# Two steps of TensorE's hand-written order moved in front of their neighbours: the state's half of a 64-row chunk's output, and one group of transposes of batch 0

## The chip, the cores and the metric

The kernel runs on one core of one Trainium2 chip. The metric is the device time of one execution in microseconds (us). The core's engines work side by side, each on its own queue of instructions: TensorE (PE in the profile, its weight loads are PEld), VectorE (DVE), ScalarE (ACT), GpSimd (POOL) and SyncE (SP), which here only starts DMAs. They are ordered against each other only by semaphores on which the kernel waits.

## The reference

Three layers follow each other. The first is an attention with a decay in place of a softmax, over 4 batches, 8 heads, 576 positions and 64 features a head; the second a feed-forward layer over the 2304 rows; the third a mixture of 8 experts, of which each row takes two. Only the first layer has to do with the change.

```python
scores = scale * np.matmul(q, k.transpose(0, 1, 3, 2))
gamma = 1.0 - 2.0 ** (-5.0 - np.arange(H, dtype=np.float32))
rel = pos[:, None] - pos[None, :]
Dmat = np.where(rel >= 0, gamma[:, None, None] ** rel[None, :, :], 0.0)
ret = scores * Dmat[None, :, :, :]
attn_out = np.matmul(ret, v)
x = attn_out.transpose(0, 2, 1, 3).reshape(B * S, H * D)
x = _moe_ref(x=x, **moe_kwargs)           # softplus(x @ w_in) @ w_out
return _moe2_ref(x=x, **moe2_kwargs)      # top-2 of 8 experts
```

## The kernel before

The 576 positions of a batch are cut into five chunks (CHUNKS), four of 128 rows and a last one of 64 (ROWS). Since the decay is a power, a chunk's output has two parts: its own scores times its values, and what all earlier chunks of the batch have left in a state (64 x 64 a head) times its queries, which are scaled by a power of the decay. The first chunk of a batch has no second part. The work of a chunk t of batch b is:

- transpose_k (L623, four instructions, one a pair of heads): TensorE turns the chunk's keys into one of three PSUM banks; keep_kT (ScalarE, L955) copies them to kTb. It waits for the keys' DMA.
- scores (L637): TensorE multiplies keys and queries into the two score banks, of which there is only one set, so it waits until both masks of the chunk before are done (scores_masked). mask_scores (VectorE, L1215, two instructions, one a bank) multiplies them by the decay and writes them to sco.
- output: first the state's part (L656; it waits for x_kept, state_kept and q_scaled), then its own part (L663; it waits for scores_masked and the values' DMA), into the same two PSUM banks. Where the chunk has 64 rows, TensorE waits between the two parts until the first has been written (x_begun). keep_x (ScalarE, L961) copies the result away (x_kept).
- add_state (L676): TensorE multiplies keys and values; VectorE adds the faded old state (L1229, or a copy, L1231, for the first chunk) and raises state_kept. The last chunk of a batch has no add_state.
- scale_k (GpSimd, L507) scales the keys once they are turned, scale_q (GpSimd, L513) the queries once their scores are made (q_scaled). For each chunk GpSimd runs scale_k of the next one and then scale_q.

Each engine's order is written out by hand. TensorE's is that of the function sequence: for chunk t it turns the keys of chunk t+1, makes the scores of t, then the output and the state of t-1. So at t = 0 of a batch it turns chunk 1's keys, makes the scores of chunk 0, and then the output of the 64-row chunk of the batch before. Batch 0 starts with its own list of steps; batches 1 and 2 run in a loop. VectorE's order is: masks of t, fade of the state (L1221), add_state of t-1. In the last batch it also rounds off pieces of the feed-forward weights (piece_rest, L1234), after t = 1, 3 and 4, and ScalarE splits them (L947). After the last batch TensorE runs ff_in(0, 0) (L712 to L714, 12 matmuls in three kinds), the output of the last batch's 64-row chunk, and ff_in(0, 1), and goes on with the feed-forward layer.

A wait written with the function alone is an instruction of its own:

```python
def alone(eng, s, count):
    if not (isinstance(count, int) and count <= 0):
        eng.wait_ge(s, count)
        eng.sem_inc(passed, 1)
```

Of the kernel before, what the change touches and what calls it, by code (L numbers as in the profile page):

```python
# [27 lines left out]
P = 128  # L28
B, H, S, DH = 4, 8, 576, 64
# [3 lines left out]
CHUNKS = -(-S // P)  # L33
ROWS = [min(P, S - t * P) for t in range(CHUNKS)]
# [71 lines left out]
def build(nc, qT, kN, vN, w_ff, w_gn, noise, w_ex, c_q, c_k, c_dec, c_sq, c_small, c_pad, out):  # L106
    with ExitStack() as ctx:
        def sem(name):
            return ctx.enter_context(nc.semaphore(name))

        def place(name, shape, dt, at):
            at = -(-at // 32) * 32
            n = 4
            for s in shape[1:]:
                n *= s
            assert BASE <= at and at + n <= nc.sbuf_usable_end, (name, at, n)
            return nc.alloc_sbuf_tensor_at(name, shape, dt, offset=at), at + n
# [16 lines left out]
        vbuf, a = place("vbuf", [P, CHUNKS, D], F32, a)  # L134
# [3 lines left out]
        state, a = place("state", [P, 2, PAIRS, DH], F32, a)  # L138
# [109 lines left out]
        x_ps = x_banks[:, :, 0:2 * P].rearrange("p e (u c) -> p e u c", u=2)  # L248
# [22 lines left out]
        ld_v = [sem(f"ld_v{t}") for t in range(CHUNKS)]  # L271
# [6 lines left out]
        scores_made, scores_masked = sem("scores_made"), sem("scores_masked")  # L278
        x_begun, x_made, x_kept = sem("x_begun"), sem("x_made"), sem("x_kept")
# [30 lines left out]
        def at_least(eng, s, count):  # L310
# [10 lines that stand above are left out]
# [10 lines left out]
        def q_of(t):  # L331

            return qbuf[:, t, 0:PAIRS * ROWS[t]].rearrange("p (h s) -> p h s", h=PAIRS)
# [272 lines left out]
        def _(pe):  # L606


            def fill(n):
                for _ in range(n):  # L610
                    pe.matmul(gate_ps[:, 0:P], zero[:, :], zero[:, :], start=True, stop=True)
# [6 lines left out]
            def transpose_k(b, t):  # L618
                r, n = ROWS[t], b * CHUNKS + t
                pe.wait_ge(ld_k[t], b * 16 + 16)  # L620
                alone(pe, kT_kept, n - BACK[t] + 1)
                for h in range(PAIRS):
                    last = pe.transpose(kT_ps[t % 3][:, h, 0:r], kbuf[0:r, t, h * P:(h + 1) * P],  # L623
                                        ident[0:r, 0:r])
                last.then_inc(kT_made, 1)

            def scores(b, t):

                r, n = ROWS[t], b * CHUNKS + t
                pe.wait_ge(kT_kept, n + 1)  # L630
                alone(pe, ld_q[t], b * 16 + 16)
                alone(pe, scores_masked, n * 2)
                q = q_of(t)
                for h in range(PAIRS):
                    for e in range(2):
                        d = slice(e * DH, (e + 1) * DH)
                        last = pe.matmul(sc_ps[e][0:r, h, 0:r], kTb[d, t % 3, h, 0:r], q[d, h, :],  # L637
                                         start=True, stop=True)
                        if h == PAIRS - 1:
                            last.then_inc(scores_made, 1)  # L640

            def output(b, t):

                r, n = ROWS[t], b * CHUNKS + t
                pe.wait_ge(scores_masked, n * 2 + 2)
                alone(pe, ld_v[t], b * 16 + 16)
                at_least(pe, x_kept, n)
                at = lambda h, e: x_ps[(h + e) % 2 * DH:((h + e) % 2 + 1) * DH, e, h // 2, 0:r]
                if t:
                    at_least(pe, state_kept, b * (CHUNKS - 1) + t)  # L650
                    alone(pe, q_scaled, b * (CHUNKS - 1) + t)
                    q = q_of(t)
                    for h in range(PAIRS):
                        for e in range(2):
                            d = slice(e * DH, (e + 1) * DH)
                            last = pe.matmul(at(h, e), state[d, (t - 1) % 2, h, :], q[d, h, :],  # L656
                                             start=(h < 2), stop=False, skip_group_check=True)
                    if r < P:
                        last.then_inc(x_begun, 1)
                        alone(pe, x_begun, b + 1)  # L660
                for h in range(PAIRS):
                    for e in range(2):
                        last = pe.matmul(at(h, e), vbuf[0:r, t, (2 * h + e) * DH:(2 * h + e + 1) * DH],  # L663
                                         sco[0:r, t % 3, e, h, 0:r], start=(t == 0 and h < 2), stop=True,
                                         skip_group_check=True)
                last.then_inc(x_made, 1)

            def add_state(b, t):

                n = b * (CHUNKS - 1) + t  # L670
                pe.wait_ge(k_scaled, n + 1)
                at_least(pe, state_kept, n)
                for h in range(PAIRS):
                    for e in range(2):
                        d = slice((2 * h + e) * DH, (2 * h + e + 1) * DH)
                        last = pe.matmul(kv_ps[e * DH:(e + 1) * DH, h, :], kbuf[:, t, d], vbuf[:, t, d],  # L676
                                         start=True, stop=True)
                last.then_inc(kv_made, 1)

            def sequence(b, first, last):  # L680

                for t in range(2 if first else 0, CHUNKS):
                    if t + 1 < CHUNKS:
                        transpose_k(b, t + 1)
                    elif not last:
                        transpose_k(b + 1, 0)
                    scores(b, t)
                    if t:
                        output(b, t - 1)
                        add_state(b, t - 1)  # L690
                    else:
                        output(b - 1, CHUNKS - 1)

            transpose_k(0, 0)
            fill(3)
# [2 lines left out]
            transpose_k(0, 1)  # L698
            fill(3)
            output(0, 0)  # L700
            scores(0, 1)
            add_state(0, 0)
            transpose_k(0, 2)
            sequence(0, True, False)
            with pe.Fori(1, B - 1) as b:
                sequence(b, False, False)
            sequence(B - 1, False, True)


            def three(o, a_hi, a_lo, b_hi, b_lo, first, last):  # L710

                pe.matmul(o, a_hi, b_hi, start=first, stop=False)  # L712
                pe.matmul(o, a_hi, b_lo, start=False, stop=False)  # L713
                return pe.matmul(o, a_lo, b_hi, start=False, stop=last)  # L714

            def ff_in(c, f):

                if f == 0 and isinstance(c, int) and c == 0:
                    pe.wait_ge(x0_lo_done, KT)
                elif f == 0:  # L720
                    pe.wait_ge(xs_lo_done, c)
                if isinstance(c, int) and c == 0:
                    pe.wait_ge(piece_lo, f + 1)
                if isinstance(c, int) and c == 0 and f == 0:
                    pe.wait_ge(kT_kept, B * CHUNKS)
                if isinstance(c, int) and c == 0 and f == 2:
                    pe.wait_ge(scores_masked, 2 * B * CHUNKS)
                at_least(pe, g_done, c * FT1 + f - 3)
                for k in range(KT):
                    w = slice(k * P, (k + 1) * P)  # L730
                    last = three(h_ps[f % 4], mw[:, f, 0, w], mw[:, f, 1, w],
                                 xs_hi[:, bass.ds(c % 2, 1), k, :].rearrange("p o n -> p (o n)"),
                                 xs_lo[:, bass.ds(c % 2, 1), k, :].rearrange("p o n -> p (o n)"),
                                 k == 0, k == KT - 1)
                last.then_inc(h_made, 1)
# [84 lines left out]
                        tile_transpose(f - (FT1 - 3), f - (FT1 - 3), 1)  # L820


            ff_in(0, 0)
            output(B - 1, CHUNKS - 1)
            ff_in(0, 1)
            pe.wait_ge(ld_small, 64)
            ff_chunk(0, False, True)
# [826 lines left out]
```

## Time and profile before

| what | value |
|---|---|
| time, median of 3 runs | 1014.98 us (1014.78 to 1015.62) |
| time of the profiled execution | 1015.1 us |
| its span, first to last instruction | 1013.3 us |
| TensorE busy | 1000.4 us, 99% of the span |
| VectorE, ScalarE, GpSimd busy | 394.9, 432.3 and 202.1 us |
| mean granted TensorE clock | 0.998 |
| attention ends on TensorE at about | 76.8 us |

The span is what the trace shows; the profiled execution's own time is 1.8 us longer, for what lies before the first and after the last instruction. The median and the profiled execution differ by 0.1 us. All start times below are us from the span's start.

### The profile page before, as it was taken

What the parts mean: (1) busy time and instruction counts of PE and PEld (TensorE: products, weight loads), DVE (VectorE), ACT (ScalarE), POOL (GpSimd) and SP (SyncE); (2) the same over time, 40 slices, a digit from 0 to 9 for tenths busy, and PEclk for the clock granted to TensorE, in tenths of its full rate; (3) what the DMA queues carried; (4) which work ended last, traced back from release to release, by engine and by line L of the source; (5) the groups of instructions that cost most, each with busy time, mean ns of one, the idle gap of its engine ahead of it and who ended that gap; (6) DMA issues with size and microseconds to landing.
All of it is one profiled execution on the core that took longest, in us unless ns stands there. A gap on an engine that the chain in (4) does not pass through costs nothing.

```text
span 1013.3 us, 21851 instructions
## 1 busy us (share of the span) xinstructions
PE 1000.4 (99%) x5932; PEld 862.8 (85%) x5933; DVE 394.9 (39%) x774; ACT 432.3 (43%) x741; POOL 202.1 (20%) x198
## 2 busy tenths in 40 slices
PE   9999999999999999999999999999999999999996
PEld 8889998998998998989878888888888888888885
DVE  3565632432432433436553222242366364222221
ACT  3347755555555455567522222232365453222221
POOL 4540000020010200200331222222222232222222
PEclk9999999999999999999999999999999999999999
DMA  8753450000000000053216222243276452211111
GB/s 272 257 170 126 135 208 1 1 32 1 1 31 0 0 31 0 22 198 125 84 36 227 63 65 66 64 156 125 86 246 237 135 176 69 66 53 53 53 48 45
DMA packets 47080, 95.33 MB, mean 94 GB/s; under 512 B 19245, under 2 KB 24749, under 8 KB 42928
## 3 DMA queue, kind: packets, MB, share of 16 engines
q1 hardware_dynamic: 24240, 66.29, 19.0%
q0 software_dynamic: 10992, 27.84, 8.7%
q10 hardware_dynamic: 11808, 0.68, 0.7%
q8 instruction: 24, 0.39, 0.2%
q14 instruction: 16, 0.13, 0.0%
HBM read 79.01 MB, written 20.37 MB: 98 GB/s over the span
## 4 chain that ended last, share of the span: by engine, by line
PE 94%; DMA 2%; issue 2%; POOL 1%; ACTq 0%; DVE 0%; ACT 0%; SPq 0%; DVEq 0%; POOLq 0%
PE bank L712 27%; PE bank L714 27%; PE bank L713 27%; PE bank L858 3%; PE bank L663 2%; PE bank L804 2%; PE bank L637 2%; PE bank L656 1%; PE bank L623 1%; PE bank L676 1%; PE bank L762 1%; DMA lists<-rec,slot 1%; DMA kdec<-c_k 1%; POOL lists L531 0%; PE bank L769 0%
## 5 line engine op out<-in xcount | busy, mean ns | idle before, releaser
L712 PE MATMUL bank<-ew,hT_hi 128*128 (+1 forms) x328 | 131.9, 402 | 1.8 <-DVE hT_lo L1464 1.8
L712 PE MATMUL bank<-ew,xgT_hi 128*128 (+1 forms) x328 | 131.9, 402 | 0.7 <-issue 0.7
L712 PE MATMUL bank<-xs_hi,mw 128*128 128x384 f32 x384 | 130.0, 339 | 0.0
L714 PE MATMUL bank<-xs_hi,mw 128*128 128x384 f32 x384 | 129.6, 337 | 0.0
L713 PE MATMUL bank<-xs_lo,mw 128*128 128x384 f32 x384 | 129.0, 336 | 0.0
L714 PE MATMUL bank<-ew,xgT_lo 128*128 (+1 forms) x328 | 128.5, 392 | 0.0
L714 PE MATMUL bank<-ew,hT_lo 128*128 (+1 forms) x328 | 128.4, 391 | 0.0
L713 PE MATMUL bank<-ew,hT_hi 128*128 (+1 forms) x328 | 127.8, 390 | 0.0
L713 PE MATMUL bank<-ew,xgT_hi 128*128 (+1 forms) x328 | 127.6, 389 | 0.0
L712 PE MATMUL bank<-mw,g_hi 128*128 128x512 f32 x288 | 114.6, 398 | 0.0
L714 PE MATMUL bank<-mw,g_lo 128*128 128x512 f32 x288 | 113.7, 395 | 0.0
L713 PE MATMUL bank<-mw,g_hi 128*128 128x512 f32 x288 | 113.5, 394 | 0.0
L1277 DVE SCALAR_TENSOR_TENSOR act_t<-bank,act_t 128x384 f32<-128x384 f32 x90 | 50.1, 557 | 160.5 <-ACT act_t L1017 159.6
L531 POOL DMA_INDIRECT lists<-rec,slot x36 | 35.7, 992 | 383.8 <-DVE slot L1368 374.6
L1107 ACT ACTIVATE hT_hi<-bank 128x512 fp32r<-128x512 f32 x82 | 44.6, 596 | 150.9 <-PE bank L858 146.9
L563 POOL DMA_INDIRECT out<-ysb,meta_y x41 | 41.9, 1021 | 280.5 <-DVE ysb L1476 280.5
L1088 ACT ACTIVATE xgT_hi<-bank 128x512 fp32r<-128x512 f32 x42 | 25.1, 597 | 140.8 <-PE bank L804 140.8
L1476 DVE SCALAR_TENSOR_TENSOR ysb<-bank,meta_y,prev 128x512 f32<-128x512 f32 x41 | 30.7, 749 | 133.1 <-PE bank L714 106.5
L1013 ACT ACTIVATE act_t<-bank 128x384 f32<-128x384 f32 x90 | 44.1, 490 | 88.8 <-PE bank L714 88.1
L1595 DVE TENSOR_TENSOR ew<-raw,ew 128x2048 f32 x24 | 55.1, 2295 | 58.9 <-ACT ew L1120 54.9
L712 PEld LDWEIGHTS bank<-xs_hi,mw 128*128 128x128 f32 x384 | 72.2, 188 | 3.9
L713 PEld LDWEIGHTS bank<-xs_lo,mw 128*128 128x128 f32 x384 | 72.1, 188 | 3.7
(191 smaller groups left out, 1654.5 us busy)
## 6 DMA issues: line engine op xcount, KB each, us to landing
raw<-w_ex SPq DMA_DIRECT2D x32, 1024.0 KB, 4.8
stage<-w_ff SPq DMA_DIRECT2D x16, 512.0 KB, 3.4
out<-blank SPq DMA_DIRECT2D x3, 1536.0 KB, 11.4
x_rows<-x2sb SPq DMA_DIRECT2D x6, 768.0 KB, 3.6
kbuf<-kN SPq DMA_DIRECT2D x16, 256.0 KB, 3.0
vbuf<-vN SPq DMA_DIRECT2D x16, 256.0 KB, 4.5
qbuf<-qT SPq DMA_DIRECT2D x15, 256.0 KB, 3.9
xg<-x_rows,meta_x POOLq DMA_INDIRECT x43, 3.4
```

Source lines behind the costliest of these rows:

```text
L531: pool.indirect_dma_start(out=lists[:, :], out_offset=bass.IndirectOffsetOnAxis(ap=slot[:, j, k:k + 1], axis=0), in_=rec[:, j, k, :], in_o ...
L563: pool.indirect_dma_start(out=out[:, :], out_offset=rows, in_=ysb[:, s, :], in_offset=None, bounds_check=N - 1, oob_is_err=False).then_inc ...
L712: pe.matmul(o, a_hi, b_hi, start=first, stop=False)
L713: pe.matmul(o, a_hi, b_lo, start=False, stop=False)
L714: return pe.matmul(o, a_lo, b_hi, start=False, stop=last)
L858: last = pe.transpose(hT_ps[k // 4][:, k % 4, :], hid[:, k * P:(k + 1) * P], ident)
L1013: nc.scalar.activation(t, h_ps[f % 4], ACT.Abs).then_inc(abs_done, 1)
L1088: nc.scalar.activation(xgT_hi[:, s, :, :], xT_ps, ACT.Copy).then_inc(xgT_hi_done, 1)
L1107: nc.scalar.activation(h_hi[:, 4 * k:4 * k + 4, :], hT_ps[k], ACT.Copy).then_inc(hT_hi_done, 1)
L1277: dve.scalar_tensor_tensor(t, h_ps[f % 4], 0.0, t, ALU.max, ALU.add).then_inc(g_done, 1)
L1476: dve.scalar_tensor_tensor(ysb[:, s, :], y_ps, meta_y[:, s, 1:2].bitcast(F32), prev[:, s, :], ALU.mult, ALU.add).then_inc(y_done, 1)
L1595: dve.tensor_tensor(part(1), raw[:, w], as32(part(0)), ALU.subtract).then_inc(w_lo_done[p], 1)
```

## The change

The function output is cut in two. output_past holds the waits for x_kept, state_kept and q_scaled and the state's part; output_own holds the waits for scores_masked, the values and x_begun and the chunk's own part. For chunks of 128 rows nothing is reordered (both are called one after the other), only the waits for the masks and the values now stand behind the state's part. For the 64-row chunk of batches 0 to 2 output_past now stands in front of the scores of the next batch's chunk 0, and output_own where output stood. For the last batch output_past stands in front of ff_in(0, 0). In batch 0, the transposes of chunk 2's keys move from behind add_state(0, 0) to in front of scores(0, 1). No instruction that computes is added or removed, and no other engine's order changes.

```diff
-            def output(b, t):
+            def output_past(b, t):
                 r, n = ROWS[t], b * CHUNKS + t
-                pe.wait_ge(scores_masked, n * 2 + 2)
-                alone(pe, ld_v[t], b * 16 + 16)
                 at_least(pe, x_kept, n)
                 if t:
                     at_least(pe, state_kept, b * (CHUNKS - 1) + t)
                     alone(pe, q_scaled, b * (CHUNKS - 1) + t)
...
                     if r < P:
                         last.then_inc(x_begun, 1)
-                        alone(pe, x_begun, b + 1)
+
+            def output_own(b, t):
+
+                r, n = ROWS[t], b * CHUNKS + t
+                pe.wait_ge(scores_masked, n * 2 + 2)
+                alone(pe, ld_v[t], b * 16 + 16)
+                if r < P:
+                    alone(pe, x_begun, b + 1)
...
+            def output(b, t):
+                output_past(b, t)
+                output_own(b, t)
...
                         transpose_k(b + 1, 0)
+                    if t == 0:
+                        output_past(b - 1, CHUNKS - 1)
                     scores(b, t)
                     if t:
                         output(b, t - 1)
                         add_state(b, t - 1)
                     else:
-                        output(b - 1, CHUNKS - 1)
+                        output_own(b - 1, CHUNKS - 1)
...
             output(0, 0)
+            transpose_k(0, 2)
             scores(0, 1)
             add_state(0, 0)
-            transpose_k(0, 2)
             sequence(0, True, False)
...
+            output_past(B - 1, CHUNKS - 1)
             ff_in(0, 0)
-            output(B - 1, CHUNKS - 1)
+            output_own(B - 1, CHUNKS - 1)
             ff_in(0, 1)
```

## Rows read from the trace of the kernel before

**Rows 1.** Page: the chain that ended last, shares of the span by engine.

```profile
PE 94%; DMA 2%; issue 2%; POOL 1%; ACTq 0%; DVE 0%; ACT 0%; SPq 0%; DVEq 0%; POOLq 0%
```

**Rows 2.** Waits of TensorE from 76 us on: total us, times, longest.

```profile
PE bank L712 <- DVE hT_lo L1464: 1.8, 2, 1.5
```

**Rows 3.** Timeline of batch 0's start: start, us, engine, line, operation [idle before].

```profile
10.09 1.16 PE L637 MATMUL bank<-qbuf,kTb 64*128 64x128 f32 x16
...
11.29 1.29 DVE L1215 TENSOR_TENSOR sco<-bank,decay 128x512 f32<-128x512 f32 x2 [2.54 <-PE bank L637]
...
12.49 0.60 ACT L955 ACTIVATE kTb<-bank 128x512 f32<-128x512 f32 x1 [3.39 <-PE bank L623]
12.54 1.04 POOL L507 TENSOR_TENSOR kbuf<-kbuf,kdec 128x512 f32<-128x512 f32 x1 [2.90 <-PE bank L623]
...
13.39 1.16 PE L637 MATMUL bank<-qbuf,kTb 64*128 64x128 f32 x16 [0.49 <-ACT kTb L955]
...
13.54 1.27 POOL L513 TENSOR_TENSOR qbuf<-qbuf,qdec 128x512 f32<-128x512 f32 x1
...
15.07 0.67 PE L656 MATMUL bank<-qbuf,state 64*64 64x128 f32 x16 [0.52 <-POOL qbuf L513]
```

**Rows 4.** The DMA of chunk 2's keys: issue at 3.5 us, us to landing.

```profile
L358 SPq DMA_DIRECT2D kbuf<-kN x1: 503/503/503, 3.5 to 3.5; - x1
...
DMA to landing us min/median/max: 5.6/5.6/5.6
```

**Rows 5.** Timeline where batch 0 passes into batch 1.

```profile
23.36 0.60 ACT L961 ACTIVATE xT<-bank 128x512 f32<-128x512 f32 x1 [1.50 <-PE bank L663]
...
23.96 0.42 DVE L1229 TENSOR_TENSOR state<-faded,bank 128x256 f32<-128x256 f32 x1 [0.94 <-PE bank L676]
...
24.29 1.16 PE L637 MATMUL bank<-qbuf,kTb 64*128 64x128 f32 x16
...
25.38 0.46 PE L656 MATMUL bank<-qbuf,state 64*64 64x64 f32 x16
25.48 1.29 DVE L1215 TENSOR_TENSOR sco<-bank,decay 128x512 f32<-128x512 f32 x2 [0.52 <-PE bank L637]
...
26.02 0.68 PE L663 MATMUL bank<-sco,vbuf 64*64 64x64 f32 x16 [0.18 <-PE bank L656]
26.64 0.66 PE L623 MATMUL bank<-square,kbuf 128*128 128x128 f32 x4
27.22 1.05 PE L637 MATMUL bank<-qbuf,kTb 64*128 64x128 f32 x14
```

**Rows 6.** Timeline of batch 1: a state's part behind its state, and the next boundary.

```profile
37.75 0.42 DVE L1229 TENSOR_TENSOR state<-faded,bank 128x256 f32<-128x256 f32 x1 [1.10 <-PE bank L676]
...
38.27 0.67 PE L656 MATMUL bank<-qbuf,state 64*64 64x128 f32 x16
...
40.67 0.42 DVE L1229 TENSOR_TENSOR state<-faded,bank 128x256 f32<-128x256 f32 x1 [1.29 <-PE bank L676]
...
40.94 1.16 PE L637 MATMUL bank<-qbuf,kTb 64*128 64x128 f32 x16
```

**Rows 7.** Timeline where attention passes into the feed-forward layer.

```profile
72.82 0.74 DVE L1215 TENSOR_TENSOR sco<-bank,decay 64x256 f32<-64x256 f32 x2
...
73.16 0.44 PE L712 MATMUL bank<-xs_hi,mw 128*128 128x384 f32 x1
...
74.02 0.42 DVE L1229 TENSOR_TENSOR state<-faded,bank 128x256 f32<-128x256 f32 x1
...
75.46 0.46 PE L656 MATMUL bank<-qbuf,state 64*64 64x64 f32 x16
...
76.10 0.68 PE L663 MATMUL bank<-sco,vbuf 64*64 64x64 f32 x16 [0.18 <-PE bank L656]
```

**Rows 8.** Timeline near the kernel's end: TensorE's longest idle time.

```profile
1000.82 0.49 PE L712 MATMUL bank<-ew,hT_hi 128*128 x1 [1.52 <-DVE hT_lo L1464]
```

**Rows 9.** Windows: busy us of each engine, granted TensorE clock, DMA.

```profile
1000.00:1003.00 3.00, 2.18 (x10) 1.82 (x11) 1.26 (x2) 0.43 (x1) 1.02 (x1) 1.00 0.25 93
```

More of the change, by code:

```diff
@@ L640, in scores, with x_at @@
                             last.then_inc(scores_made, 1)
-            def output(b, t):
+            def x_at(h, e, r):
+                return x_ps[(h + e) % 2 * DH:((h + e) % 2 + 1) * DH, e, h // 2, 0:r]
+            def output_past(b, t):
                 r, n = ROWS[t], b * CHUNKS + t
-                pe.wait_ge(scores_masked, n * 2 + 2)
-                alone(pe, ld_v[t], b * 16 + 16)
                 at_least(pe, x_kept, n)
-                at = lambda h, e: x_ps[(h + e) % 2 * DH:((h + e) % 2 + 1) * DH, e, h // 2, 0:r]
                 if t:
@@ L655, in output @@
                             d = slice(e * DH, (e + 1) * DH)
-                            last = pe.matmul(at(h, e), state[d, (t - 1) % 2, h, :], q[d, h, :],
+                            last = pe.matmul(x_at(h, e, r), state[d, (t - 1) % 2, h, :], q[d, h, :],
                                              start=(h < 2), stop=False, skip_group_check=True)
@@ L659, in output @@
                         last.then_inc(x_begun, 1)
-                        alone(pe, x_begun, b + 1)
+            def output_own(b, t):
[4 more added lines that the diff above has]
+                    alone(pe, x_begun, b + 1)
                 for h in range(PAIRS):
                     for e in range(2):
-                        last = pe.matmul(at(h, e), vbuf[0:r, t, (2 * h + e) * DH:(2 * h + e + 1) * DH],
+                        last = pe.matmul(x_at(h, e, r), vbuf[0:r, t, (2 * h + e) * DH:(2 * h + e + 1) * DH],
                                          sco[0:r, t % 3, e, h, 0:r], start=(t == 0 and h < 2), stop=True,
```

## The prediction

> **What bounds the kernel now.** I read the page's chain first: 94% of the span is TensorE's [rows 1]. Time that TensorE gains or loses in attention therefore reaches the end, if nothing behind it swallows the difference. The view of TensorE's waits behind attention says that little can: the largest entry is two waits for VectorE of 1.8 us in all [rows 2], of which 1.5 us lie at 1000.8 us [rows 8], for something made from TensorE's own output there. A shift of TensorE at 77 us is a shift of the end.
>
> Then I read the timeline of the three places that the edit touches. In batch 0's start TensorE stands idle twice: 0.49 us in front of the scores of chunk 1's successor, put down to ScalarE's copy of chunk 2's keys, and 0.52 us in front of the first state's part, put down to GpSimd's scaling of the queries [rows 3]. Where a batch passes into the next, there is one gap of 0.18 us between the two parts of the 64-row chunk's output [rows 5], the wait for x_begun; it comes back behind the last batch [rows 7] and at the other two boundaries.
>
> **The change part by part.** No computing instruction is added or removed, so all is in waits.
>
> *Price of a wait.* The new waits are for VectorE. In batch 1 a state ends at 37.75 + 0.42 = 38.17 and TensorE's matmul on it starts at 38.27 [rows 6]: 0.10 us from the end of VectorE's record to TensorE's start. The same distance from ScalarE is 12.49 + 0.60 = 13.09 to 13.39, 0.30 us [rows 3]. I take 0.10, being the same kind of wait on the same engine, and keep 0.30 as the upper bound.
>
> *Chunk 2's keys one group sooner.* Their DMA is issued at 3.5 and lands 5.6 us later, at 9.1 [rows 4]; the transposes would now start at 10.09 [rows 3], so there is 1.0 us of cover. A group of transposes takes 27.22 - 26.64 = 0.58 us [rows 5]. The scores of chunk 1 slip by that from 10.09 to 10.67. Now ScalarE's copy is long done when the scores of chunk 2 want it, but another wait is right behind it: those scores also need both masks of chunk 1, because there is one set of score banks. The masks begin 1.20 us after the scores and last 1.29 us together [rows 3]: 11.87 to 13.16, and with 0.10 the scores of chunk 2 start at 13.26 instead of 13.39. So of the 0.49 us wait only 0.13 goes; the rest is now VectorE's. The second wait does go: GpSimd's scaling of the keys started 12.54 - 11.29 = 1.25 us after the masks because the transposes were behind them; now the transposes end at 10.67, it runs to about 11.9 (1.04 us long), and the queries' scaling of 1.27 us [rows 3] ends near 13.2. The state's part can follow the scores at once, 25.38 - 24.29 = 1.09 us after their start [rows 5]: 14.35 instead of 15.07. Gain: 0.72 us. Bounds: with 0.30 for the wait on the masks the gain is 0.52; at most 1.0, the two idle times together.
>
> *Boundaries of batches 0, 1 and 2.* The state's part now follows the transposes, where the scores started at 24.29. But it needs the state of the chunk before, which VectorE ends at 23.96 + 0.42 = 24.38 [rows 5]; keep_x has ended earlier, at 23.96. So it starts at 24.48. The state's part of 64 rows takes 0.46 us [rows 5], the scores of the next batch start at 24.94, 0.65 later than before. The gap in front of the own part is gone, because the scores now lie between. That would bring TensorE back to even: scores 1.09, own part 26.64 - 26.02 = 0.62 and transposes 0.58 end at 27.23, where the next scores started at 27.22. What is late next is the mask. Before, the scores of chunk 1 followed those of chunk 0 after 2.93 us; now only 2.29 us of work lie between. The masks begin 1.19 us after the scores' start (25.48 - 24.29) and take 1.29 [rows 5]; with 0.10 that is 2.58 us. The scores of chunk 1 start at 24.94 + 2.58 = 27.52 instead of 27.22: 0.30 us lost. Queued behind this wait is all that TensorE still has for the batch, and VectorE and ScalarE wait for that, so nothing catches up. At the next boundary the state ends at 40.67 + 0.42 = 41.09 against a start of the scores at 40.94 [rows 6], 0.15 us behind and not 0.09: 0.36 lost. The third I take like the second. Sum: 0.30 + 0.36 + 0.36 = 1.02 us lost. Bounds: if the masks do not bind (their cost then is nothing), the three cost 0.01 + 0.07 + 0.07 = 0.15; with 0.30 for each of the two waits, 0.4 more each, 2.2 us.
>
> *Behind the last batch.* Before, ff_in(0, 0) started right behind add_state at 73.16 and covered the time in which VectorE made the last state, which ends only at 74.02 + 0.42 = 74.44 [rows 7], since the masks in front of it start at 72.82 and end at 73.56. Now the state's part stands in front of ff_in and nothing covers it: it starts at 74.54, TensorE idle for 1.38 us. Then come the state's part, 0.46, so ff_in at 75.00, and the own part 75.46 - 73.16 = 2.30 us later, at 77.30 instead of 76.10: 1.20 us lost, of which the 0.18 gap gained back is already taken off. Bounds: 1.1 if the refill behind the wait is shorter, 1.4 with 0.30 for the wait.
>
> **The sum** is -0.72 + 1.02 + 1.20 = +1.50 us on the profiled execution's 1015.1 us (span 1013.3 and 1.8 around it); on the median of 1014.98, 1016.5 us. That is 0.15% slower; about 0.2%, 2.0 us, is what a measurement of this kernel can tell from no change.
>
> **The rivals.**
>
> *Each wait on VectorE costs what the one on ScalarE costs.* Eight waits enter the sum (one at the start, two at each boundary, one at the end). At 0.30 instead of 0.10 each, 1.6 us come on top: +3.1, 1018.1 us. For it speaks that a wait made with alone is followed by another instruction; against it, that the row of 0.10 has the same wait behind it. It decides from 0.17 us a wait: 1.50 + 8 x 0.07 = 2.06 us, over the bound.
>
> *The stall behind the last batch is hidden anyway*, if the feed-forward layer has slack of its own. Against it speaks the view of the waits, which has no wait of TensorE there [rows 2]. It would give 1.50 - 1.20 = +0.3, 1015.3 us.
>
> *The masks do not bind at the boundaries*: +1.50 - 0.87 = +0.6, 1015.6 us. The bound is close, 2.58 against 2.29 us of work.
>
> *The producers are ready earlier than I say* and the change gives only its gains, 0.72 at the start and four gaps of 0.18: 1013.5 us. The state's end at 74.44 speaks against it.
>
> *TensorE's clock falls in the 1.38 us stall.* In the trace TensorE stood idle for 1.52 us in front of 1000.82 [rows 8], and the granted clock of that window is 1.00 [rows 9], the level of 2.4 GHz. If it did fall, the 3.4 us of work that follow (0.46 + 2.30 + 0.62) would take twice as long: +4.9, 1019.9 us. The Trainium skill ("TensorE: Matmul & The Clock Gate", Part 1: The HAM clock gate) says that TensorE's default is the throttled clock and that only sustained activity releases it, which speaks against any order that leaves it idle; the trace has a longer pause that did not cost it. By that page alone the rival would deserve more than I give it.
>
> **How the numbers follow.** Forecast 0.61 (its own range 1015.8 to 1017.3), dearer waits 0.17, hidden stall at the end 0.09, masks not binding 0.08, gains only 0.03, clock 0.02. Range 1015.2 to 1018.0 us: it leaves out the two last and the outer edges of the others. Slower by over 0.2% holds the dearer waits, the clock and the forecast's upper edge: 0.22. Faster by over 0.2% would need more than even the gains-only case gives: 0.03. Within 0.2%: 0.75.
>
> **What would show it.** After the change: TensorE's 0.52 us wait for GpSimd near 15 us gone, the state's part there near 14.35; the wait in front of the scores at 13.3 put down to VectorE's masks. At each boundary a state's part at 0.1 us behind VectorE's state, the own part without its gap, and then a new gap near 0.3 us in front of the scores of chunk 1, ended by L1215. Near 73.5 us (all of attention having moved by -0.72 + 1.02 = +0.3) an idle time of TensorE of about 1.4 us, ended by L1229, and ff_in behind it. The forecast is wrong if that last idle time is missing or much shorter, or if the gaps at the boundaries are 0.2 us wider.

## The result and the profile after

The changed kernel took 1018.29 us (median of 13 runs, 1016.35 to 1020.01) against 1014.89 us (13 runs, 1014.0 to 1017.06). The ratio is 1.0025 with a 95% interval of 1.0017 to 1.0034, about 2.5 us slower. That is on the far side of the forecast of +1.5 us (1016.5): the changed kernel's median lies 0.3 us above the range's upper end of 1018.0, and the ratio applied to 1014.98 gives 1017.5, inside it. In the terms of the prediction it is slower by over 0.2%, the outcome that had a chance of 0.22 against 0.75 for one within 0.2%, though the interval reaches down to 0.17%. The two profiled executions differ by more, 1018.29 against 1015.1 us and a span of 1016.5 against 1013.3.

The waits of TensorE over the whole span (releaser: us in total, times, longest) show the new entries. Lines from 639 on have moved: L656 is now L657, L663 is L671, L676 is L688, L712 is L726, L1215 is L1230, L1229 is L1244.

```profile
PE bank L657 <- DVE state L1244: 1.7, 3, 1.3
PE bank L726 <- DVE hT_lo L1479: 1.7, 2, 1.5
PE bank L637 <- issue: 1.5, 1, 1.5
...
PE bank L637 <- DVE sco L1230: 1.0, 4, 0.3
```

The waits for GpSimd and ScalarE at the start, 0.52 and 0.49 us in [rows 3], and the four gaps of 0.18 us, as in [rows 5], are gone. In their place TensorE waits for VectorE's state (1.7 us; the third boundary's 0.2 us is put down to issue) and for its masks (1.0 us, four times: once at the start and once at each boundary). The third line is something else: a wait for nothing that the profile shows.

The timeline of the start (compare [rows 3]):

```profile
10.51 1.16 PE L637 MATMUL bank<-qbuf,kTb 64*128 64x128 f32 x16
...
11.70 1.29 DVE L1230 TENSOR_TENSOR sco<-bank,decay 128x512 f32<-128x512 f32 x2 [3.26 <-PE bank L637]
...
13.13 1.16 PE L637 MATMUL bank<-qbuf,kTb 64*128 64x128 f32 x16 [0.26 <-DVE sco L1230]
...
14.22 0.67 PE L657 MATMUL bank<-qbuf,state 64*64 64x128 f32 x16
```

This execution had started its first output 0.17 us sooner (8.90 against 9.07 us). The rest of the way from 15.07 to 14.22 us, 0.68 us, is the gain. The scores of chunk 2 gained only 0.09 us of it (13.39 to 13.13, less the 0.17).

The first boundary (compare [rows 5]), from the transposes in front of it to the scores of chunk 1:

```profile
22.86 0.66 PE L623 MATMUL bank<-square,kbuf 128*128 128x128 f32 x4
...
23.12 0.42 DVE L1244 TENSOR_TENSOR state<-faded,bank 128x256 f32<-128x256 f32 x1 [0.94 <-PE bank L688]
...
23.69 0.46 PE L657 MATMUL bank<-qbuf,state 64*64 64x64 f32 x16 [0.17 <-DVE state L1244]
...
24.20 1.21 PE L637 MATMUL bank<-qbuf,kTb 64*128 64x128 f32 x16
25.34 0.55 PEld L671 LDWEIGHTS bank<-sco,vbuf 64*64 64x64 f32 x16
...
25.37 1.29 DVE L1230 TENSOR_TENSOR sco<-bank,decay 128x512 f32<-128x512 f32 x2 [1.25 <-PE bank L637]
...
26.80 1.16 PE L637 MATMUL bank<-qbuf,kTb 64*128 64x128 f32 x16 [0.19 <-DVE sco L1230]
```

The own part stands right behind the scores, without its gap. But the state's part starts 0.15 us after VectorE's record of the state ends (23.54), and the scores of chunk 1 start 0.14 us after the record of the masks ends (26.66). From the transposes to the scores of chunk 1 it takes 3.94 us. Before it took 23.70 to 27.22, 3.52 us. So this boundary loses 0.42 us; the other two, measured in the same way, lose 0.48 and 0.42.

Behind the last batch (compare [rows 7]):

```profile
74.67 0.63 PE L688 MATMUL bank<-vbuf,kbuf 128*64 128x64 f32 x16
...
76.08 0.42 DVE L1244 TENSOR_TENSOR state<-faded,bank 128x256 f32<-128x256 f32 x1
...
76.60 0.46 PE L657 MATMUL bank<-qbuf,state 64*64 64x64 f32 x16 [1.30 <-DVE state L1244]
...
76.99 0.44 PE L726 MATMUL bank<-xs_hi,mw 128*128 128x384 f32 x1
```

TensorE stands idle for 1.30 us until the state is there. ff_in follows it, and the own part starts at 79.28, 4.61 us after add_state. Before it was 72.60 to 76.10, 3.50 us. The place costs 1.11 us.

And this lies in the middle of the scores of chunk 4 of batch 1, where nothing was changed:

```profile
37.16 0.62 PE L637 MATMUL bank<-qbuf,kTb 64*64 64x64 f32 x13
...
39.23 0.33 PE L637 MATMUL bank<-qbuf,kTb 64*64 64x64 f32 x3 [1.46 <-issue]
39.44 0.46 PEld L657 LDWEIGHTS bank<-qbuf,state 64*64 64x64 f32 x16
```

Thirteen of the sixteen matmul records of one group run, then TensorE stops for 1.46 us, then the last three run. No semaphore stands inside the group. What follows, the state's part, has its first weight load 2.29 us after the group's (37.15 to 39.44) where it was 0.67 us before (37.57 to 38.24), so the stop costs 1.62 us. The waits that were forecast, -0.68 + 0.42 + 0.48 + 0.42 + 1.11 = +1.75, the stop, and the 0.17 us by which the first output was sooner add up to 1.75 + 1.62 - 0.17 = 3.2 us, the difference of the two spans. The question for the runs was which of this belongs to the change.

### The profile page after: what moved, and what is told of

Its sections match the earlier page's. It is cut to its first block, busy times and chain, and to the rows that moved or that the text cites. A ratio compares the mean times of both kernels' runs of the same rounds, so it can differ in the third digit from the quotient of the medians.

```text
span 1016.5 us, 21854 instructions
## 1 busy us (share of the span) xinstructions
PE 1000.9 (98%) x5932; PEld 863.0 (85%) x5933; DVE 395.5 (39%) x774; ACT 432.5 (43%) x741; POOL 201.9 (20%) x198
## 4 chain that ended last, share of the span: by engine, by line
PE 88%; DMA 2%; issue 1%; POOL 1%; ACTq 0%; DVE 0%; ACT 0%; DVEq 0%; POOLq 0%; SPq 0%
PE bank L726 27%; PE bank L728 27%; PE bank L727 27%; PE bank L873 3%; PE bank L818 2%; PE bank L776 1%; DMA lists<-rec,slot 1%; POOL lists L531 0%; PE bank L783 0%; DMA xg<-x_rows,meta_x 0%; DMA prev<-out,meta_y 0%; DMA out<-ysb,meta_y 0%; PE bank L791 0%; PE bank L911 0%; ACTq L345 0%
## 5 line engine op out<-in xcount | busy, mean ns | idle before, releaser
L726 PE MATMUL bank<-ew,hT_hi 128*128 (+1 forms) x328 | 131.9, 402 | 1.7 <-DVE hT_lo L1479 1.7
L726 PE MATMUL bank<-ew,xgT_hi 128*128 (+1 forms) x328 | 131.9, 402 | 0.7 <-issue 0.7
L726 PE MATMUL bank<-xs_hi,mw 128*128 128x384 f32 x384 | 130.0, 338 | 0.0
L726 PE MATMUL bank<-mw,g_hi 128*128 128x512 f32 x288 | 114.6, 398 | 0.0
L531 POOL DMA_INDIRECT lists<-rec,slot x36 | 35.8, 994 | 384.9 <-DVE slot L1383 375.7
L726 PEld LDWEIGHTS bank<-xs_hi,mw 128*128 128x128 f32 x384 | 72.2, 188 | 3.9
```

What stands on the lines that cost most here:

```text
L531: pool.indirect_dma_start(out=lists[:, :], out_offset=bass.IndirectOffsetOnAxis(ap=slot[:, j, k:k + 1], axis=0), in_=rec[:, j, k, :], in_o ...
```

## The experiments

For the attention of each run I give the time on TensorE from its first output of batch 0 to the own part of the last 64-row chunk: it leaves out how early the first loads land and all that comes behind. It was 67.0 us before and 70.4 us in the changed kernel's profile.

**The three edits alone.** Only the early transposes:

```diff
             output(0, 0)
+            transpose_k(0, 2)
             scores(0, 1)
             add_state(0, 0)
-            transpose_k(0, 2)
```

> Only the transposes of batch 0's chunk 2 are moved in front of scores(0, 1); the 64-row chunk's output stays in one piece where it stood. Theory A (the waits on VectorE explain everything but a stop of 1.5 us in the middle of batch 1's scores of chunk 4): 0.7 us faster than before, 1014.3 us, the wait for GpSimd near 15 us gone, 0.26 us left in front of the scores of chunk 2. Theory B (the stop in batch 1 comes from the start being earlier against the loads): the stop of about 1.5 us is here too, and the time is 0.8 us slower than before, 1015.8 us.

Measured: 0.9993 of the kernel before (0.9983 to 1.0002), so the 0.7 us of theory A in size, with an interval that just holds 1. The attention took 67.5 us, with TensorE idle for 1.06 us at the same place of batch 1 in it, as theory B had it: each theory has half of what was seen. The wait on the masks at the start is there as forecast and no other, and the state's part there starts 5.33 us after the first output (14.71 us against 9.38), before 6.00: 0.67 us gained.

```profile
12.70 0.66 PE L623 MATMUL bank<-square,kbuf 128*128 128x128 f32 x4
13.62 1.16 PE L637 MATMUL bank<-qbuf,kTb 64*128 64x128 f32 x16 [0.26 <-DVE sco L1227]
14.71 0.67 PE L657 MATMUL bank<-qbuf,state 64*64 64x128 f32 x16
```

Only the three boundaries:

```diff
+                    if t == 0:
+                        output_past(b - 1, CHUNKS - 1)
                     scores(b, t)
...
-                        output(b - 1, CHUNKS - 1)
+                        output_own(b - 1, CHUNKS - 1)
```

> Only the three boundaries inside the batches: the state's part of the 64-row chunk stands in front of the next batch's first scores. Theory A: each boundary loses 0.4 to 0.5 us (0.5 for the state's part, 0.1 to 0.2 for the state, the rest for the masks), 1.3 us together, 1016.2 us. Rival (masks don't bind, the gap of 0.18 us gained pays for the state's wait): 0.2 us slower, 1015.1 us. If the stop in batch 1 hangs on the loop's code being laid out anew, it is here too, and the time is 2.8 us over before.

Measured: 1.0015 (1.0003 to 1.0026). The attention took 69.2 us, again with a stop, of 0.8 us idle. The time fits theory A (1.3 us forecast, 1.5 measured). The first boundary goes from transposes at 23.63 to scores at 27.57, 3.94 us as in the changed kernel.

Only the state's part in front of ff_in:

```diff
+            output_past(B - 1, CHUNKS - 1)
             ff_in(0, 0)
-            output(B - 1, CHUNKS - 1)
+            output_own(B - 1, CHUNKS - 1)
```

> Only the state's part of the last 64-row chunk is moved in front of ff_in(0, 0). Theory A: TensorE is idle for 1.3 us until VectorE has made the last state, and the time is 1.2 us over before, 1016.1 us. Rival (the stall is hidden by what follows): no change, 1014.9 us. No stop in the middle of batch 1, since neither the code nor the times in front of it have changed.

Measured: 1.0016 (1.0007 to 1.0025), attention 68.5 us. The wait for the state is 1.30 us as in the changed kernel. My last sentence was wrong: this kernel has exactly the order of the kernel before up to the last batch, and still stops for a short time at the same instruction of batch 1 (two weight loads 0.51 us apart that are 0.01 us apart in the kernel before). So the stop does not need the changed order. It costs 1.21 us in e1_start, 0.93 in e2_bounds and 0.39 here, measured as the 1.62 above. Without it the three attentions are 0.7 us shorter, 1.3 longer and 1.1 longer than before, together +1.7: the three edits add up to the +1.75 of the places.

**The changed kernel again, unaltered.**

> The changed kernel once more, unaltered, for a second trace. If the stop of 1.5 us in the middle of batch 1's scores of chunk 4 belongs to this program, it is in this trace too, at the same instruction, and the time is 3.3 us over before. If it is a matter of single executions, it is gone or elsewhere, and the span is 1.5 us shorter than 1016.5.

Measured: 1.0021 (1.0011 to 1.0032). Its list of TensorE's waits holds VectorE's state (1.9 us, four times), its masks (1.0 us, four times), and none put down to issue in the scores. The stop is almost gone, but not wholly. The weight loads of that group take longer than in the kernel before (first this trace, then the kernel before):

```profile
37.26 0.76 PEld L637 LDWEIGHTS bank<-qbuf,kTb 64*64 64x64 f32 x16 [0.17 <-issue]
```

```profile
37.57 0.54 PEld L637 LDWEIGHTS bank<-qbuf,kTb 64*64 64x64 f32 x16 [0.17 <-issue]
```

The longer time lies between the 13th and the 14th load, the place of the stop, which are 0.23 us apart here; what follows comes 0.11 us later by it. The attention took 68.9 us, 1.9 more than before. The span was 1016.2 us and not 1.5 us shorter, because another 1.1 us had gone behind attention. It is in the windows (busy us of each engine, granted TensorE clock, DMA share, GB/s); for the kernel before, the window of 504 to 508 us has a clock of 1.00 and 25 matmul records.

```profile
498.00:504.00 6.00, 6.00 (x44) 5.58 (x43) 2.38 (x4) 3.69 (x8) 1.04 (x1) 0.99 0.83 175
504.00:508.00 4.00, 4.00 (x12) 3.11 (x12) 2.20 (x18) 2.20 (x4) 0.00 (x0) 0.59 0.01 3
508.00:512.00 4.00, 4.00 (x26) 3.47 (x25) 1.36 (x11) 2.85 (x5) 0.00 (x0) 1.00 0.01 2
```

At about 504 us the granted clock fell to its lower level of 1.2 GHz for most of the window, and the same weight loads took 0.33 us instead of 0.19: seven of them follow each other after 0.43 us instead of 0.23, and with the two at the edges about 1.6 us are lost. Shortly in front of the fall TensorE had run 24 products of only 16 columns (L896 of the kernel before, 2.6 us long). It fell so in 5 of the 13 traces of this study, e3_end and this one among them, somewhere between 501 and 504 us; the other eight have the same 24 products and no fall, so the products alone do not bring it about, and what does is open. The mean clock listed for each execution tells the two kinds apart: 0.996 in the five traces, 0.998 or 0.999 in the eight. It was 0.997 or less in 33 of the 91 executions of the kernel before that were timed beside the runs, and in 15 of the 37 of the changed kernel. So the fall is not made by the edit, and hardly more frequent with it.

**The stop in batch 1.** In the traces, the program is fetched in packets of 16 KB on a DMA queue of its own. One of them starts shortly in front of this place; that it is the one with the code for it is an inference from the times:

| trace | packet starts, us | the 14th weight load follows the 13th after, us |
|---|---|---|
| before | 34.9 | 0.01 |
| e4_again | 35.4 | 0.23 |
| e3_end | 35.8 | 0.51 |
| e7_halfmask | 36.3 | 0.78 |
| e6_gap | 36.5 | 1.05 |
| e1_start | 36.6 | 1.33 |
| e2_bounds | 37.0 | 1.05 |
| changed kernel | 37.0 | 1.73 |

The stop always falls between the same two weight loads. How long it is depends also on when TensorE gets there, but the second load comes 2.2 to 2.4 us after the packet's start in all seven traces that stop. In the kernel before, 2.4 us after the packet's start is 37.3 us, and the load was due only at 37.9. The Trainium skill ("Runtime: NRT & Kernel Launch", Instruction fetch mechanics) says that an engine's code comes in blocks of 16 KB on a DMA queue that its sequencer drives, and that crossing a block is mostly hidden. The packets agree with the first; for the second, the trace has a stop of 1.46 us. To see whether the data loaded just then makes the block late, I moved the two 512 KB pieces of weights:

```diff
-                if b == 1:
+                if b == 2:
                     load_piece(0, 0)
                     load_piece(1, 1)
```

> The kernel before, with one change on the DMA side: the two 512 KB pieces of feed-forward weights are loaded behind batch 2's loads instead of behind batch 1's, so that they don't move while TensorE's code for the end of batch 1 is fetched. Theory A (TensorE stops at one and the same instruction of batch 1 when the 16 KB block of code with it arrives late behind data): in the trace the block is fetched at 35 us or sooner and there is no stop; the times lose part of their upper cluster, median 0.5 to 1 us under the kernel before. Rival (the block's arrival has nothing to do with these loads): the block can still come at 36 to 37 us, and the times are those of before.

Measured, on the kernel before: 1.0005 (0.9994 to 1.0016), so the 0.5 to 1 us that theory A expected did not come. In its trace the block starts at 33.3 us and there is no stop, attention 67.1 us; the kernel before had none in its own trace either. The same edit on the changed kernel:

> The changed kernel with the two pieces of weights loaded behind batch 2, so that no stop falls into batch 1. Theory (waits on VectorE cost 1.8 us net, the stop is extra): attention takes 68.8 to 69.0 us on TensorE from its first output to its last, 1.8 to 1.9 more than before, and the code's block comes at 33 to 34 us. Rival (the stop goes with the changed order): a stop at the same instruction again.

Measured: 1.0018 (1.0009 to 1.0027), block at 34.0 us, no stop, attention 69.0 us, 1.9 more than before, all as forecast. The ratio lies within the intervals of the two runs without this edit, so what the stop costs in time is read from the traces alone. The windows from 28 to 38 us show what the edit takes away (first the changed kernel run again, then with the pieces moved; the first number behind the clock is the DMA share):

```profile
28.00:38.00 10.00, 10.00 (x190) 8.78 (x188) 6.02 (x12) 3.31 (x6) 4.88 (x4) 1.00 0.95 293
```

```profile
28.00:38.00 10.00, 10.00 (x194) 8.75 (x192) 6.17 (x12) 3.04 (x6) 5.02 (x5) 1.00 0.67 195
```

Of the eight traces with the pieces behind batch 1, seven stop there; of the five with the pieces behind batch 2, none.

**Are the masks part of a boundary's cost?** In the changed kernel, chunk 0 of batches 1 to 3 masks half the pairs only:

```diff
-                    mask_scores(b, t)
+                    mask_scores(b, t, PAIRS if first or t else PAIRS // 2)
```

> The changed kernel with VectorE masking only half the heads' scores in chunk 0 of batches 1 to 3 (the other half of the scores there is left out, so the attention of those chunks is incomplete). Theory A (a boundary's cost of 0.45 us is 0.15 us of waiting for the state and 0.3 us of waiting for the masks): the wait in front of the scores of chunk 1 is gone, a boundary takes 3.6 to 3.7 us from its transposes to the scores of chunk 1, against 3.52 before and 3.95 changed. Rival (the cost is a price of TensorE itself, for the changed order of shapes): it stays at 3.9.

Measured, from its trace alone (span 1016.6 us, with the stop, the two loads 0.78 us apart, and the halved clock in it): the wait on the masks is gone.

```profile
23.35 0.66 PE L623 MATMUL bank<-square,kbuf 128*128 128x128 f32 x4
...
24.18 0.46 PE L657 MATMUL bank<-qbuf,state 64*64 64x64 f32 x16 [0.17 <-DVE state L1244]
...
24.69 1.21 PE L637 MATMUL bank<-qbuf,kTb 64*128 64x128 f32 x16
...
25.85 0.76 DVE L1230 TENSOR_TENSOR sco<-bank,decay 128x256 f32<-128x256 f32 x2 [1.24 <-PE bank L637]
...
27.03 1.16 PE L637 MATMUL bank<-qbuf,kTb 64*128 64x128 f32 x16
```

The boundary takes 3.68 us, between the 3.52 before and the 3.94 changed: 0.26 us of its loss was the masks', and 0.16 us remains. It comes with the wait on the state, 0.17 us by the row. At the second boundary it is 3.77 us against 3.52 and 4.00. The rival's 3.9 did not come.

**A version that keeps the gain.** If the masks need about 2.6 us from scores to scores, the gap in front of the own part must be covered without making that distance shorter. So the state's part goes back behind the scores, and the own part behind the next transposes. ScalarE's and VectorE's split of the first rows, which needs that own part, moves from chunk 0 to chunk 2:

```diff
                     elif not last:
                         transpose_k(b + 1, 0)
+                    if t == 1:
+                        output_own(b - 1, CHUNKS - 1)
                     scores(b, t)
...
                     else:
-                        output(b - 1, CHUNKS - 1)
+                        output_past(b - 1, CHUNKS - 1)
...
-                    if t == (CHUNKS - 1 if first else 0):
+                    if t == (CHUNKS - 1 if first else 2):
```

> The early transposes of batch 0 kept, the state's part of the 64-row chunk back behind the next batch's first scores, and its own part moved behind the next transposes (chunk 2's keys), which then cover the gap of 0.18 us; ScalarE's and VectorE's split of the first rows moves from chunk 0 to chunk 2 of each batch to stay out of the masks' way. Theory A (the masks need 2.6 us from scores to scores, here 2.75 us of work lie between): the boundaries gain 0.1 to 0.2 us each, no wait on a mask, 0.4 us on top of the 0.7 of the early transposes, 1.1 us under the kernel before where TensorE's code isn't late. Rival (any rearrangement there ends in a new wait): as e1_start or slower.

Measured: 1.0002 (0.9993 to 1.0012), so the forecast gain of 1.1 us does not show in the time. Its trace has a stop in batch 1 (the loads 1.05 us apart) and the halved clock from 502 us; the boundary itself did what was forecast:

```profile
23.74 0.66 PE L623 MATMUL bank<-square,kbuf 128*128 128x128 f32 x4
...
24.32 1.16 PE L637 MATMUL bank<-qbuf,kTb 64*128 64x128 f32 x16
...
25.42 0.46 PE L657 MATMUL bank<-qbuf,state 64*64 64x64 f32 x16
25.52 1.29 DVE L1229 TENSOR_TENSOR sco<-bank,decay 128x512 f32<-128x512 f32 x2 [0.52 <-PE bank L637]
25.81 0.66 PE L623 MATMUL bank<-square,kbuf 128*128 128x128 f32 x4
26.39 0.68 PE L671 MATMUL bank<-sco,vbuf 64*64 64x64 f32 x16
...
27.01 1.16 PE L637 MATMUL bank<-qbuf,kTb 64*128 64x128 f32 x16
```

No wait, and 3.27 us instead of 3.52. With the pieces moved as well:

> All that helped together: the early transposes, the own part behind the next transposes with the splits moved, and the pieces of weights loaded behind batch 2. Theory A: no stop in batch 1, attention ends 1.2 us sooner than in the kernel before, and the time is 1 to 1.5 us under it, 1014.9 us for a median before of 1016.2. Rival: as for e5 and e6, the same as before.

Measured: 0.9993 (0.9984 to 1.0002), 0.7 us where 1 to 1.5 were forecast, span 1011.7, attention 65.6 us, 1.4 less than before, and no stop. The interval still held 1, so I ran it again:

> The same kernel as e8_best, timed once more because 0.9993 with an interval up to 1.0002 left open whether it beats the kernel before. Theory (its attention is 1.4 us shorter on TensorE and nothing behind it changes): ratio 0.998 to 0.999, its interval below 1. Rival (the single executions' halved clock and late code drown it): the interval holds 1 again.

Measured: 0.9981 (0.9972 to 0.9989), attention 65.6 us again. The two sets of the same kernel give 0.7 and 1.9 us; the 1.4 us of the traces lies between them. Its profiled execution had the halved clock, span 1013.3. Last, on top of it, the end:

```diff
-            ff_in(0, 0)
-            output(B - 1, CHUNKS - 1)
+            ff_in(0, 0, range(KT - 1))
+            output_past(B - 1, CHUNKS - 1)
+            ff_in(0, 0, range(KT - 1, KT))
+            output_own(B - 1, CHUNKS - 1)
```

> As e8_best, and behind the last batch the state's part of the 64-row chunk stands in front of the last quarter of ff_in(0, 0), at about 75 us in the times of the kernel before, when its state is ready (74.4), so that the quarter covers the gap in front of the own part. Theory (0.18 us of gap gained, one more change of shape paid): 0 to 0.15 us under e8_best's attention. Rival (the state is late here too): a wait for L1229's copy in front of it and a longer attention.

Measured: 0.9981 (0.9972 to 0.9991), span 1011.3, attention 65.5 us: no wait for the state, and as good as nothing gained on top. The start of the state's part comes 0.27 us behind the last ff_in matmul in front of it (73.52 to 73.79, where the next ff_in matmul would come after 0.17); that the second change of shape eats the covered gap fits this row, and was not tested by itself.

## Why the prediction was right, and where it was short

**The chain and its end.** That a shift of TensorE in attention is a shift of the end held: from the last own part to the end of the span it was 937.2 us before and after. That the two agree so well is luck: over the eight traces without the fall of the clock this stretch takes 936.0 to 937.2 us, whatever the edit, and over the five with it 938.1 to 938.5.

**The early transposes.** Forecast a gain of 0.72 us, measured 0.68 and alone 0.67. The step that counted was the wait behind the named one: the profile put 0.49 us down to ScalarE's copy, but taking that away gained 0.09 (forecast 0.13), because VectorE's masks came next. The trace after names them, with 0.26 us.

**The boundaries.** Forecast 0.30, 0.36 and 0.36, measured 0.42, 0.48 and 0.42. That the masks bind is shown by e7_halfmask, where halving them takes their wait away; that the state does is read from the row that names it. The term mis-sized is the price of a wait on VectorE: I took 0.10 us from its record's end to TensorE's start, from one row of batch 1; after the change it is 0.15 and 0.14 at the first boundary and 0.14 in front of the scores at the start (12.99 to 13.13). It is 0.10 for the last state (76.50 to 76.60), so it is not one price for all waits on VectorE; why it differs no run shows. The other small part is that the scores follow the state's part 0.51 us after its start and not 0.46.

**The end.** Forecast 1.20, measured 1.11, with a stall of 1.30 where I had 1.38. The rival that it would be hidden fell: alone, the edit costs 1.0016 (1.0007 to 1.0025).

**The sum.** Forecast +1.50. By the places of the trace it is +1.75 on TensorE, and the attention of the two other traces of this order is 1.9 us longer (68.9, with 0.1 of stop in it, and 69.0 against 67.0 us); by the measured times 1.0025, 1.0021 and 1.0018 in three sets of runs, 2.5, 2.1 and 1.8 us. Dearer waits, the rival on the slower side, decides from 0.17 us a wait as I had worked out, 0.56 us over eight waits. The waits were dearer by 0.05 us at most, some 0.3 us in all, so on TensorE the outcome lies about midway between my forecast and the 2.06 us from which this rival decides. Whether the time is over 0.2% longer is not settled by these intervals. The mechanism was right; that the sum came within 0.3 us owes something to the end, which was 0.09 us cheaper than forecast while the boundaries were 0.30 us dearer.

**What I had not seen** are the late block of code and the fall of the clock between 501 and 507 us. Each moves a single execution by up to 1.6 us, as much as the change itself. The first explains why one pair of profiled executions shows 3.2 us; neither of the two has the second. That the changed order makes a late block likelier is not excluded, since the kernel before was traced once only, with its block 0.5 us sooner than the smallest stop needs; that it is not needed for it is shown by e3_end. The rival of a clock falling in the 1.3 us stall fell: the granted clock of 72 to 80 us is 1.00. The Trainium skill ("TensorE: Matmul & The Clock Gate", Part 1: The HAM clock gate) has the chip set the clock by how busy TensorE has been lately; this case's traces show that a pause of 1.3 us did not bring it down (granted clock 1.00), and that it fell in five of them where TensorE's records have no pause (6.00 of 6.00 us busy from 498 to 504 us in e4_again), so they neither confirm nor refute it.

## What to carry to other kernels

When a wait is to be removed, work out the next one at the same place before counting its length as a gain: with one set of score banks, the masks here need 2.6 us from scores to scores, and work taken from between them below that comes back as a wait. Work that waits for another engine's last result should stand behind other work and not in front of it; here 2.3 us of ff_in had covered a state that comes 1.3 us late. A change worth 1 us in 1000 can't be read off one pair of traces: compare the same stretch in several, and look for stops inside a group that has no semaphore.

## What the runs showed of the hardware that was not expected

TensorE stopped at one and the same weight load in seven of eight traces, for 0.2 to 1.7 us from one load to the next, when a 16 KB packet of code started at 35.4 us or later; the load came 2.2 to 2.4 us after the packet's start each time. The DMA engines were 84 to 95% busy from 28 to 38 us in all eight; with the data moved (67 to 73%) the packet started at 33.2 to 34.0 us and there was no stop in five traces. In 5 of 13 traces the granted clock fell to 1.2 GHz for a few us between 501 and 507 us, not long behind a group of 24 matmuls of 16 columns that all 13 have, and it did not fall in an idle stretch of 1.3 us. The time from the end of VectorE's record to the start of the TensorE matmul that waits for it was 0.14 us for the masks and 0.10 to 0.15 us for the state.
